# Interleaving the two layers of the expert stage, with the block loop written out for two blocks

## The chip, the cores and the metric

One core of one Trainium2 chip runs the whole program. The metric is the device time of one execution in microseconds (us). Engines: PE (TensorE matmuls; PEld its weight loads), DVE (VectorE), ACT (ScalarE), POOL (GpSimd), SP (SyncE). A name with q behind it (PEldq, DVEq, ACTq, POOLq) is the instruction sequencer of that engine, which does register work, branches and waits and hands the other instructions to the engine.

## The reference, cut to what matters

```
def _moe2_ref(x, modality_id, w_gate, modality_bias, w1, w2):
    logits = x @ w_gate + modality_bias[modality_id]
    e_idx = np.argmax(logits, axis=1)
    ...
    for e in range(E):                      # E = 8 experts, N = 3072 tokens, D = 512, F = 1024
        mask = e_idx == e
        h = np.maximum(x[mask] @ w1[e], 0.0)
        out[mask] = gate_w[mask, None] * (h @ w2[e])

def reference(...):
    attn_out = _attn_ref(q, k, v, n_sink, window)        # sink and window attention
    x = attn_out as (3072, 512)
    x = _moe_ref(x, w_in, w_out)                         # h = x @ w_in; (h - tanh(h)) @ w_out
    return _moe2_ref(x, ...)                             # the stage that is changed
```

## The kernel before

The program has two parts. The first, "front", does attention, the dense layer and the gate, writes the tokens to device memory (x2) and a table of slots per expert, and ends near 830 us. The second, "experts", is the one that is changed. It works on blocks of 128 tokens of one expert. A plan made on the chip gives the number of blocks (the data of this run make 25, numbered 0 to 24), the row of slots of each block, its turn (which expert of the order, row 1 of the table `meta`) and, in `meta_late`, at which block the weights of a next turn are looked over, scaled and split. Here only one such change of weights happens, in blocks 0 to 2.

Products are made in float16 with both factors split in a high and a low part, three products for each. A block j passes these steps; the line numbers are those of the profile.

- `load_slots`, `gather` (POOL, L1543, L1550): the slots of block j+2 and then its 128 rows of x, in one buffer `xg`, free again when block j+1 is transposed. A one-element addition on POOL (L97) carries their waits.
- `scale_x` (DVE L1562 to L1566, ACT L1569): a power-of-two scale for each token.
- `transpose_x` (PE L1577 into `xt_ps`, ACT L1582 to `xg_hi`, DVE L1585 to `xg_lo`).
- `hidden` (PE L1602): 8 f x 3 products x 4 k = 96 products of 128 columns into two banks `hid_ps`; the weights of the turn's parity are addressed through registers, computed line by line. Then ACT (L1611) `hid_hi`, DVE (L1614) `hid_lo`, for each half.
- `output` (PE L1646): 8 f x 3 = 24 products of 512 columns into `y_ps`; ACT (L1652) scales by `y_scale` (DVE L1629, L1632, after ACT's load of the slots, L1622); POOL (L1657) scatters `y` to the output.
- `look_ahead`, `scale_ahead`, `split_ahead`: the weights of the next turn. Each asks `meta_late` by a read into a register (`read`, L1499) and an If, on PE once for a block, on DVE four times, on ACT three times, also where there is nothing to do.

The order on each engine is the order of the calls in `iteration`. PE does hidden(j), the question of `scale_ahead`, the transposes of j+1, output(j). Blocks 0 and 1 are written out, and then one loop runs j from 2 to NB-1 = 37 and skips by an If what lies behind the last block.

Of the kernel before, what the change touches and what calls it, by code (L numbers as in the profile page):

```python
# [16 lines left out]
F32 = mybir.dt.float32  # L17
# [33 lines left out]
MB = NB + 2  # L51
# [1413 lines left out]
def experts(nc, dram, shared):  # L1465
# [5 lines left out]
    with ExitStack() as ctx:  # L1471
# [9 lines left out]
        xg_hi, xg_lo = (sb(n, [P, DM], F16) for n in ("xg_hi", "xg_lo"))  # L1481
        hid_hi, hid_lo = (sb(n, [P, FE], F16) for n in ("hid_hi", "hid_lo"))
        y_scale = sb("y_scale", [P, 1], F32)
# [4 lines left out]
        y_ps = ps("y_ps", [P, DM], F32)  # L1488
# [3 lines left out]
                 "hid_mm hid_hi hid_lo y_mm y_step y_set y_out scattered slot_y_in "  # L1492
# [33 lines left out]
        def split_ahead(E, eng, j, at, pieces):  # L1526
            if at is not None and E in ("act", "dve") and len(pieces):
                s = read(eng, 2, at, NE)
                with eng.If(s > 0):
                    eng.wait_ge(q["y_mm"], j)  # L1530
                    shared.split(E, eng, s, pieces)
# [21 lines left out]
        def scale_x(E, eng, j):  # L1553

            if E == "dve":
                step = chain(eng, q["x_step"], 4 * j)
                ts = eng.tensor_scalar
                eng.wait_ge(q["gathered"], 16 * (j + 1))
                need(eng, q["x_scaled"], j)
                if not (isinstance(j, int) and j < 2):  # L1560
                    eng.wait_ge(q["y_set"], j - 1)
# [4 lines left out]
                ts(column(x_undo, j % 2).bitcast(I32), x_exp[:], float(-EXP1), None, ALU.add).then_inc(q["x_set"], 1)  # L1566
# [4 lines left out]
        def transpose_x(E, eng, j):  # L1571

            if E == "pe":
                eng.wait_ge(q["x_scaled"], j + 1)
                need(eng, q["xt_lo"], j)
                for k in range(KD):
                    mm = eng.transpose(xt_ps[:, k * P:(k + 1) * P], xg[:, k * P:(k + 1) * P], ident[:])  # L1577
                mm.then_inc(q["xt_done"], 1)
            if E == "act":
                eng.wait_ge(q["xt_done"], j + 1)  # L1580
                need(eng, q["hid_mm"], 2 * j)
                eng.activation(xg_hi[:], xt_ps[:, :], ACT.Copy).then_inc(q["xt_hi"], 1)  # L1582
            if E == "dve":
                eng.wait_ge(q["xt_hi"], j + 1)
                eng.tensor_tensor(xg_lo[:], xt_ps[:, :], xg_hi[:], ALU.subtract).then_inc(q["xt_lo"], 1)  # L1585

        def hidden(E, eng, j, s):

            for c in range(2):
                if E == "pe":  # L1590
                    par = s % 2
                    if c == 0:
                        eng.wait_ge(q["xt_lo"], j + 1)
                    if not (isinstance(j, int) and j == 0):
                        eng.wait_ge(q["hid_lo"], 2 * j - 1 + c)
                    for f in range(4 * c, 4 * c + 4):
                        i = 0
                        for x, w in ((xg_lo, shared.hi), (xg_hi, shared.lo), (xg_hi, shared.hi)):
                            for k in range(KD):
                                if c == 0 and f == 0 and i < KD:  # L1600
                                    eng.wait_ge(shared.w_lo[k], s + 1)
                                mm = eng.matmul(hid_ps[c][:, (f - 4 * c) * P:(f - 4 * c + 1) * P],  # L1602
                                                shared.piece(w, k, par)[:, f * P:(f + 1) * P], x[:, k * P:(k + 1) * P],
                                                start=(i == 0), stop=(i == 3 * KD - 1))
                                i += 1
                    mm.then_inc(q["hid_mm"], 1)
                half = slice(c * 512, (c + 1) * 512)
                if E == "act":
                    eng.wait_ge(q["hid_mm"], 2 * j + c + 1)
                    need(eng, q["y_mm"], j)  # L1610
                    eng.activation(hid_hi[:, half], hid_ps[c][:, :], ACT.Relu).then_inc(q["hid_hi"], 1)  # L1611
                if E == "dve":
                    eng.wait_ge(q["hid_hi"], 2 * j + c + 1)
                    eng.scalar_tensor_tensor(hid_lo[:, half], hid_ps[c][:, :], 0.0, hid_hi[:, half], ALU.max, ALU.subtract)\  # L1614
                       .then_inc(q["hid_lo"], 1)
# [8 lines left out]
        def output_scale(E, eng, j, s):  # L1624

            if E == "dve":
                eng.wait_ge(q["slot_y_in"], 16 * (j + 1))
                need(eng, q["y_out"], j)
                eng.tensor_tensor(y_scale[:], slot_y[:, 1:2].bitcast(F32), column(x_undo, j % 2), ALU.mult)\  # L1629
                   .then_inc(q["y_step"], 1)  # L1630
                eng.wait_ge(q["y_step"], j + 1)
                eng.tensor_tensor(y_scale[:], y_scale[:], column(shared.undo, s), ALU.mult).then_inc(q["y_set"], 1)  # L1632

        def output(E, eng, j, s):

            if E == "pe":
                par = s % 2
                need(eng, q["y_out"], j)
                for f in range(KF):
                    if f % 4 == 0:  # L1640
                        eng.wait_ge(q["hid_lo"], 2 * j + f // 4 + 1)
                    if f % 2 == 0:
                        eng.wait_ge(shared.w_lo[KD + f // 2], s + 1)
                    for i, (l, w) in enumerate(((hid_lo, shared.hi), (hid_hi, shared.lo), (hid_hi, shared.hi))):
                        rhs = shared.piece(w, KD + f // 2, par)[:, (f % 2) * DM:(f % 2 + 1) * DM]
                        mm = eng.matmul(y_ps[:, :], l[:, f * P:(f + 1) * P], rhs, start=(f == 0 and i == 0),  # L1646
                                        stop=(f == KF - 1 and i == 2))
                mm.then_inc(q["y_mm"], 1)
            if E == "act":
                eng.wait_ge(q["y_mm"], j + 1)  # L1650
                eng.wait_ge(q["y_set"], j + 1)
                eng.activation(y[:], y_ps[:, :], ACT.Copy, scale=y_scale[:]).then_inc(q["y_out"], 1)  # L1652
            if E == "pool":
                eng.wait_ge(q["y_out"], j + 1)
# [6 lines left out]
        def iteration(E, eng, j, ago_1, ago_2):  # L1661

            turn = 0 if isinstance(j, int) and j == 0 else read(eng, 1, j, NE) if E in ("pe", "dve") else None
# [24 lines left out]
            if E == "pool":  # L1688
                load_slots(E, eng, j + 2)
                gather(E, eng, j + 2)  # L1690
                output(E, eng, j, turn)

        def program(E, eng):
# [13 lines left out]
            scale_x(E, eng, 0)  # L1707
            transpose_x(E, eng, 0)
# [4 lines left out]
            scale_x(E, eng, 1)  # L1713
# [6 lines left out]
            if E == "pool":  # L1720
                eng.wait_ge(q["gathered"], 16 * (last + 3))
                eng.wait_ge(q["scattered"], 16 * (last + 1))
# [76 lines left out]
```

## Time and profile before

| what | value |
|---|---|
| median of 3 runs | 1199.46 us (1196.58 to 1199.63) |
| the profiled execution | 1196.78 us, its span 1195.0 us |
| busy in the span | PE 1048.7, DVE 731.0, ACT 620.8, POOL 401.1 us |
| granted TensorE clock, mean over the span | 0.964 |

The span goes from the first to the last instruction of the profiled execution. PE is busy for 88% of it; ends of matmuls are modelled, so that the starts of neighbouring matmuls say more about their rate than the busy time does.

### The profile page before, as it was taken

What the parts mean: (1) busy time and instruction counts of PE and PEld (TensorE: products, weight loads), DVE (VectorE), ACT (ScalarE), POOL (GpSimd) and SP (SyncE); (2) the same over time, 40 slices, a digit from 0 to 9 for tenths busy, and PEclk for the clock granted to TensorE, in tenths of its full rate; (3) what the DMA queues carried; (4) which work ended last, traced back from release to release, by engine and by line L of the source; (5) the groups of instructions that cost most, each with busy time, mean ns of one, the idle gap of its engine ahead of it and who ended that gap; (6) DMA issues with size and microseconds to landing.
All of it is one profiled execution on the core that took longest, in us unless ns stands there. A gap on an engine that the chain in (4) does not pass through costs nothing. (4 is left out here: it accounts for less than half of the span.)

```text
span 1195.0 us, 27235 instructions
## 1 busy us (share of the span) xinstructions
PE 1048.7 (88%) x7844; PEld 684.4 (57%) x7845; DVE 731.0 (61%) x2392; ACT 620.8 (52%) x1422; POOL 401.1 (34%) x463
## 2 busy tenths in 40 slices
PE   1767898999999999999999999982699999999995
PEld 0534455665665665665665665541466667666763
DVE  6787977678878678878678655565462222222221
ACT  2776766666677666676666664451342222222221
POOL 4786774223254124254124211002232222222221
PEclk9968999999999999999999999996799999999998
DMA  9821112313212412212312100400411111011111
GB/s 295 262 66 32 33 45 68 95 32 65 57 32 39 137 32 50 73 32 36 87 32 37 54 2 10 159 1 27 168 44 37 43 36 44 27 44 35 44 35 34
DMA packets 24248, 74.18 MB, mean 62 GB/s; under 512 B 10016, under 2 KB 10016, under 8 KB 22624
## 3 DMA queue, kind: packets, MB, share of 16 engines
q1 hardware_dynamic: 14768, 59.66, 18.4%
q0 software_dynamic: 5792, 13.43, 3.5%
q8 instruction: 42, 0.69, 0.3%
q10 hardware_dynamic: 3600, 0.03, 0.2%
q14 instruction: 46, 0.38, 0.1%
HBM read 60.04 MB, written 13.33 MB: 61 GB/s over the span
## 5 line engine op out<-in xcount | busy, mean ns | idle before, releaser
L758 PE MATMUL acc<-w_out_all,g_hi 128*128 128x512 f16 x768 | 228.3, 379 | 0.0
L702 PE MATMUL h_ps<-xt_hi,w_in_all 128*128 128x384 f16 x1024 | 210.4, 328 | 16.3 <-DVE g_raw L723 16.3
L758 PE MATMUL acc<-w_out_all,g_lo 128*128 128x512 f16 x384 | 145.4, 379 | 3.2 <-DVE g_lo L743 1.7
L702 PEld LDWEIGHTS h_ps<-xt_hi,w_in_all 128*128 128x128 f16 x1024 | 97.6, 98 | 76.7 <-DVE g_raw L723 14.7
L590 ACT ACTIVATE pt_hi<-pt_ps 128x256 f16<-128x256 f32 (+2 forms) x224 | 83.4, 379 | 109.5 <-PE pt_ps L607 105.0
L97 POOL TENSOR_TENSOR tick<-tick 1x1 f32<-1x1 f32 x87 | 17.2, 198 | 349.9 <-DVE payload L878 113.5
L743 DVE SCALAR_TENSOR_TENSOR g_lo<-g_raw,batch_scale,g_hi 128x384 f16<-128x384 f32 x128 | 95.1, 743 | 33.1 <-ACT g_hi L733 30.7
L758 PEld LDWEIGHTS acc<-w_out_all,g_hi 128*128 128x128 f16 x768 | 74.9, 98 | 69.2
L714 ACT ACTIVATE g_raw<-h_ps,batch_scale 128x384 f32<-128x384 f32 x128 | 74.2, 579 | 75.0 <-PE h_ps L702 73.8
L594 DVE TENSOR_TENSOR pt_lo<-pt_ps,pt_hi 128x256 f16<-128x256 f32 (+2 forms) x224 | 94.3, 423 | 28.9 <-ACT pt_hi L590 27.5
L428 POOL TENSOR_TENSOR q_stack<-qk_raw,q_stack 64x768 f16<-64x768 f32 x31 | 50.8, 1638 | 165.6 <-ACT q_stack L424 165.6
L702 PE MATMUL h_ps<-xt_lo,w_in_all 128*128 128x384 f16 x512 | 105.5, 329 | 0.0
L571 ACT ACTIVATE normed<-probs,row_sum 128x260 f32<-128x260 f32 (+1 forms) x192 | 92.9, 484 | 19.7 <-DVE row_sum L566 19.6
L723 DVE SCALAR_TENSOR_TENSOR g_raw<-h_ps,batch_scale,g_raw 128x384 f32<-128x384 f32 x128 | 78.4, 612 | 39.8 <-ACT g_raw L714 38.7
L733 ACT ACTIVATE g_hi<-g_raw,batch_scale 128x384 f16<-128x384 f32 x128 | 78.0, 610 | 43.6 <-DVE g_raw L723 43.1
L1602 PE MATMUL hid_ps<-xg_hi,ew_lo 128*128 128x128 f16 x800 | 95.8, 219 | 0.0
L553 ACT ACTIVATE probs<-probs,neg_max 128x260 f32<-128x260 f32 (+1 forms) x192 | 92.7, 483 | 5.8 <-DVE neg_max L548 5.7
L428 POOL TENSOR_TENSOR kl_stack<-qk_raw,kh_stack 128x1048 f16<-128x1048 f32 (+1 forms) x31 | 60.1, 1939 | 99.1 <-ACT kh_stack L424 97.9
L607 PE MATMUL pt_ps<-ident,normed 128*128 128x128 f32 x352 | 74.1, 286 | 20.4 <-ACT normed L571 20.4
L1614 DVE SCALAR_TENSOR_TENSOR hid_lo<-hid_ps,hid_hi 128x512 f16<-128x512 f32 x50 | 34.3, 691 | 91.8 <-ACT hid_hi L1611 91.8
L548 DVE CUSTOM_DVE_ANT_0 probs<-s_ps,mask 128x260 f32<-128x260 f32 (+1 forms) x180 | 73.1, 406 | 23.7 <-issue 22.4
L1602 PE MATMUL hid_ps<-xg_lo,ew_hi 128*128 128x128 f16 x800 | 85.1, 222 | 1.5 <-DVE xg_lo L1585 1.5
(263 smaller groups left out, 2222.0 us busy)
## 6 DMA issues: line engine op xcount, KB each, us to landing
qk_raw<-in_qk SPq DMA_DIRECT2D x64, 454.0 KB, 6.1
raw<-in_w SPq DMA_DIRECT2D x16, 512.0 KB, 8.5
v_raw<-in_v SPq DMA_DIRECT2D x4, 1536.0 KB, 9.8
x_tokens<-x SPq DMA_DIRECT2D x24, 256.0 KB, 4.8
w_in_all<-in_w_in SPq DMA_DIRECT2D x4, 1024.0 KB, 13.0
w_out_all<-in_w_out SPq DMA_DIRECT2D x4, 1024.0 KB, 12.2
slot_g<-slots POOLq DMA_DIRECT2D x27, 1.0 KB, 2.0
xg<-x_tokens,slot_g POOLq DMA_INDIRECT x27, 3.4
```

The lines of the kernel that those rows point to most:

```text
L428: eng.tensor_tensor(lo, raw[half], hi[half], ALU.subtract).then_inc(q["conv_lo"], 1)
L553: eng.activation(probs[:, r, cols], probs[:, r, cols], ACT.Exp, bias=neg_max[:, r:r + 1], scale=-1.0, accum_out=row_sum[:, r:r + 1]).then_ ...
L571: eng.activation(normed[:, u % 6, cols], probs[:, r, cols], ACT.Copy, scale=row_sum[:, r:r + 1])\
L590: eng.activation(pt_hi[:, at, :], out, ACT.Copy).then_inc(q["pt_hi_done"], 1)
L594: eng.tensor_tensor(pt_lo[:, at, :], out, pt_hi[:, at, :], ALU.subtract).then_inc(q["pt_lo_done"], 1)
L702: mm = eng.matmul(h_ps, w16[0][:, f, x * DM + k * P:x * DM + (k + 1) * P], r[:, par, k, :], start=(i == 0), stop=(i == 3 * KD - 1))
L714: eng.activation(g_raw[:, f % 2, :], h_ps, ACT.Tanh, scale=batch_scale[:, b, 0:1]).then_inc(q["tanh_done"], 1)
L723: eng.scalar_tensor_tensor(g, h_ps, batch_scale[:, b, 0:1], g, ALU.mult, ALU.subtract).then_inc(q["g_done"], 1)
L733: eng.activation(g_hi[f % 2][:], g, ACT.Copy, scale=batch_scale[:, b, 1:2]).then_inc(q["g_hi_done"], 1)
L743: eng.scalar_tensor_tensor(g_lo[f % 2][:], g, batch_scale[:, b, 1:2], g_hi[f % 2][:], ALU.mult, ALU.subtract)\
L758: mm = eng.matmul(acc[t][:, :], l[f % 2][:, t * P:(t + 1) * P], w16[1][:, f, x * DM:(x + 1) * DM], start=(f == 0 and i == 0), stop=(f == N ...
L1602: mm = eng.matmul(hid_ps[c][:, (f - 4 * c) * P:(f - 4 * c + 1) * P], shared.piece(w, k, par)[:, f * P:(f + 1) * P], x[:, k * P:(k + 1) * P ...
```

## The change

Iteration j now makes hidden(j) and output(j-1) together: after each of the 24 products of 512 columns come 4 of the 96 small ones. The question of `scale_ahead` and the transposes of block j+1 come after the 14th of the 24. `y_ps`, `xg_hi` and `xg_lo` get a second buffer, `relu` of the second half of block j moves into iteration j+1, the scale of the output is made in two steps (`output_part`, and `output_scale` at the end of DVE's iteration), and `scale_x` of block j+1 comes at the start of iteration j instead of that of j+2 near its end. PE reads two turns for a block, that of j and that of j-1. The loop is written out for two blocks in an inner loop of four trips, inside an outer loop of five; a whole trip of the outer loop is skipped behind the last block. Block 0's first layer and the last block's second layer stand alone (`first_iteration`, `last_output`).

```
-MB = NB + 2
+MB = NB + 6
...
-        xg_hi, xg_lo = (sb(n, [P, DM], F16) for n in ("xg_hi", "xg_lo"))
+        xg_hi, xg_lo = ([sb(f"xg_{n}{i}", [P, DM], F16) for i in range(2)] for n in ("hi", "lo"))
...
-        y_ps = ps("y_ps", [P, DM], F32)
+        y_ps = [ps(f"y_ps{i}", [P, DM], F32) for i in range(2)]
...
+        def turn_of(eng, j):
+            return 0 if isinstance(j, int) and j == 0 else read(eng, 1, j, NE)
+
+        def products(eng, j, p, free, ago_1):
+
+            turn = turn_of(eng, j)
+            before = turn_of(eng, j - 1)
+            small = hidden_products(eng, j, p, turn)
+            for i, _ in enumerate(output_products(eng, j - 1, 1 - p, free, before)):
+                if i == 14:
+                    scale_ahead("pe", eng, ago_1)
+                    transpose_x("pe", eng, j + 1, 1 - p)
+                for _ in range(4):
+                    next(small)
+
+        def iteration(E, eng, j, p, ago_1, ago_2):
+
             if E == "pe":
-                hidden(E, eng, j, turn)
-                scale_ahead(E, eng, ago_1)
-                transpose_x(E, eng, j + 1)
-                output(E, eng, j, turn)
-            if E == "act":
-                hidden(E, eng, j, turn)
-                transpose_x(E, eng, j + 1)
-                load_slots_again(E, eng, j)
+                products(eng, j, p, 0 if ago_2 is None else j - 2, ago_1)
+            if E == "act":
+                relu(E, eng, j - 1, 1)
+                scale_x(E, eng, j + 1, 1 - p)
+                relu(E, eng, j, 0)
+                transpose_x(E, eng, j + 1, 1 - p)
+                load_slots_again(E, eng, j - 1)
                 split_ahead(E, eng, j, ago_2, range(KD, PIECES))
                 look_ahead(E, eng, j)
-                split_ahead(E, eng, j, ago_1, range(2))
-                output(E, eng, j, turn)
-                scale_x(E, eng, j + 2)
-                split_ahead(E, eng, j, ago_1, range(2, KD))
-            if E == "dve":
-                hidden(E, eng, j, turn)
-                transpose_x(E, eng, j + 1)
-                output_scale(E, eng, j, turn)
+                split_ahead(E, eng, j, ago_1, range(KD))
+                output(E, eng, j - 1, 1 - p)
+            if E == "dve":
+                relu(E, eng, j - 1, 1)
+                output_part(E, eng, j - 1, 1 - p, turn_of(eng, j - 1))
+                scale_x(E, eng, j + 1, 1 - p)
+                scale_ahead(E, eng, ago_1)
+                relu(E, eng, j, 0)
+                transpose_x(E, eng, j + 1, 1 - p)
                 split_ahead(E, eng, j, ago_2, range(KD, PIECES))
                 look_ahead(E, eng, j)
-                scale_ahead(E, eng, ago_1)
-                scale_x(E, eng, j + 2)
                 split_ahead(E, eng, j, ago_1, range(KD))
+                output_scale(E, eng, j - 1)
...
-            iteration(E, eng, 0, None, None)
-            iteration(E, eng, 1, 0, None)
-            with eng.Fori(2, NB) as j:
-                with eng.If(j <= last):
-                    iteration(E, eng, j, j - 1, j - 2)
...
+            first_iteration(E, eng)
+            iteration(E, eng, 1, 1, 0, None)
+            with eng.Fori(0, (NB + 5) // 8) as g:
+                with eng.If(8 * g + 2 <= last):
+                    with eng.Fori(4 * g + 1, 4 * g + 5) as i:
+                        j = 2 * i
+                        with eng.If(j <= last):
+                            iteration(E, eng, j, 0, j - 1, j - 2)
+                            with eng.If(j + 1 <= last):
+                                iteration(E, eng, j + 1, 1, j, j - 1)
+            last_output(E, eng, last)
```

## Rows read from the trace of the kernel before

**Rows 1.** The page: busy time of each engine; one instruction queue (packets, MB).

```profile
PE 1048.7 (88%) x7844; PEld 684.4 (57%) x7845; DVE 731.0 (61%) x2392; ACT 620.8 (52%) x1422; POOL 401.1 (34%) x463
...
q8 instruction: 42, 0.69, 0.3%
```

**Rows 2.** The chain that ended last, expert stage: start us, us, what.

```profile
856.23 7.04 PE y_ps L1646 x24
...
891.49 6.77 PE hid_ps L1602 x96
...
1037.08 6.50 PE hid_ps L1602 x96
1043.58 0.84 issue
1044.42 0.63 PE xt_ps L1577 x4
1045.05 5.18 PE y_ps L1646 x24
...
1169.13 6.59 PE hid_ps L1602 x96
```

**Rows 3.** Windows, PE alone, of one block's small products: stretch, length, busy (count), clock.

```profile
1050.05:1052.72 2.67, 2.67 (x49) 1.00 0.00 0
1052.98:1056.90 3.92, 3.82 (x47) 1.00 0.18 67
```

**Rows 4.** PE's sequencer by line, 1044.5 to 1057.7: count, ns min/median/max, first and last start.

```profile
L1646 PEldq FUSED_REGOPS  x8: 46/46/46, 1044.6 to 1046.6; - x8
L1717 PEldq COMPARE_BRANCH  x1: 208/208/208, 1046.9 to 1046.9; - x1
L1718 PEldq COMPARE_BRANCH  x1: 82/82/82, 1047.3 to 1047.3; - x1
L1499 PEldq TENSOR_LOAD <-meta x1: 297/297/297, 1047.6 to 1047.6; - x1
L1595 PEldq FUSED_REGOPS  x1: 42/42/42, 1048.3 to 1048.3; - x1
L1602 PEldq FUSED_REGOPS  x32: 46/46/94, 1048.5 to 1055.8; - x32
L1602 PEldq ALU_OP  x32: 32/32/32, 1049.0 to 1056.3; - x32
L1522 PEldq COMPARE_BRANCH  x1: 215/215/215, 1057.1 to 1057.1; - x1
```

**Rows 5.** Timeline of the block of rows 4 on ACT and DVE: start us, us, what [idle before].

```profile
1045.81 0.69 DVE L1585 TENSOR_TENSOR xg_lo<-xt_ps,xg_hi 128x512 f16<-128x512 f32 x1 [0.87 <-ACT xg_hi L1582]
...
1051.18 0.69 DVE L1562 TENSOR_REDUCE x_top<-xg 128x1 f32<-128x512 f32 x1 [2.85 <-issue]
...
1052.82 0.72 ACT L1569 ACTIVATE xg<-xg,x_scale 128x512 f32<-128x512 f32 x1 [1.87 <-DVE x_undo L1566]
```

**Rows 6.** The DMA answer of the whole span, issues: count, KB each, us to landing.

```profile
slot_g<-slots POOLq DMA_DIRECT2D x27, 1.0 KB, 2.0
xg<-x_tokens,slot_g POOLq DMA_INDIRECT x27, 3.4
...
out<-y,slot_y POOLq DMA_INDIRECT x25, 2.8
```

**Rows 7.** Timeline of the first blocks on DVE.

```profile
852.70 0.69 DVE L1562 TENSOR_REDUCE x_top<-xg 128x1 f32<-128x512 f32 x1 [8.15 <-DMA xg<-x_tokens,slot_g]
...
859.36 4.60 DVE L1319 TENSOR_REDUCE tops<-raw 128x1 f32<-128x1024 f32 x4 [0.68 <-issue]
...
880.41 4.94 DVE L1373 SCALAR_TENSOR_TENSOR ew_lo<-raw,ew_scale,ew_hi 128x1024 f32 x4 [0.95 <-issue]
```

**Rows 8.** The end: the last output and scatter.

```profile
1182.40 0.69 ACT L1652 ACTIVATE y<-y_ps,y_scale 128x512 f32<-128x512 f32 x1 [4.49 <-PE y_ps L1646]
...
1183.95 1.02 POOL L1657 DMA_INDIRECT out<-y,slot_y  x1 [0.60 <-issue]
```

**Rows 9.** DVE's sequencer at the loop's branch, 1176 to 1196.

```profile
L1717 DVEq COMPARE_BRANCH  x14: 50/56/56, 1185.7 to 1194.6; - x14
```

**Rows 10.** Windows, PE alone, around the first gap of the stage, with the granted clock.

```profile
852.40:854.90 2.50, 0.24 (x5) 1.00 0.36 138
854.90:856.20 1.30, 0.66 (x4) 1.00 0.01 0
856.20:857.50 1.30, 1.27 (x5) 0.69 0.01 0
857.50:858.50 1.00, 1.00 (x4) 0.50 0.39 58
```

**Rows 11.** The DMA answer from 1090 to 1120 us: all queues that moved anything.

```profile
q0 software_dynamic: 432, 1.25, 12.9%
q10 hardware_dynamic: 288, 0.00, 0.5%
```

More of the change, by code:

```diff
@@ L1580, in transpose_x @@
                 eng.wait_ge(q["xt_done"], j + 1)
-                need(eng, q["hid_mm"], 2 * j)
-                eng.activation(xg_hi[:], xt_ps[:, :], ACT.Copy).then_inc(q["xt_hi"], 1)
+                if not (isinstance(j, int) and j < 2):
+                    eng.wait_ge(q["hid_mm"], 2 * j - 2)
+                eng.activation(xg_hi[p][:], xt_ps[:, :], ACT.Copy).then_inc(q["xt_hi"], 1)
             if E == "dve":
                 eng.wait_ge(q["xt_hi"], j + 1)
-                eng.tensor_tensor(xg_lo[:], xt_ps[:, :], xg_hi[:], ALU.subtract).then_inc(q["xt_lo"], 1)
@@ L1587, in hidden, with hidden_products @@
-        def hidden(E, eng, j, s):
+                eng.tensor_tensor(xg_lo[p][:], xt_ps[:, :], xg_hi[p][:], ALU.subtract).then_inc(q["xt_lo"], 1)
+        def hidden_products(eng, j, p, s):
+            par = s % 2
+            eng.wait_ge(q["xt_lo"], j + 1)
             for c in range(2):
[L1590 to L1607, printed above, removed]
-                if E == "act":
-                    eng.wait_ge(q["hid_mm"], 2 * j + c + 1)
-                    need(eng, q["y_mm"], j)
-                    eng.activation(hid_hi[:, half], hid_ps[c][:, :], ACT.Relu).then_inc(q["hid_hi"], 1)
-                if E == "dve":
-                    eng.wait_ge(q["hid_hi"], 2 * j + c + 1)
-                    eng.scalar_tensor_tensor(hid_lo[:, half], hid_ps[c][:, :], 0.0, hid_hi[:, half], ALU.max, ALU.subtract)\
-                       .then_inc(q["hid_lo"], 1)
@@ new lines, in hidden_products @@
+                if not (isinstance(j, int) and j == 0):
+                    eng.wait_ge(q["hid_lo"], 2 * j - 1 + c)
+                for f in range(4 * c, 4 * c + 4):
+                    i = 0
+                    for x, w in ((xg_lo, shared.hi), (xg_hi, shared.lo), (xg_hi, shared.hi)):
+                        for k in range(KD):
+                            if f == 0 and i < KD:
+                                eng.wait_ge(shared.w_lo[k], s + 1)
+                            mm = eng.matmul(hid_ps[c][:, (f - 4 * c) * P:(f - 4 * c + 1) * P],
+                                            shared.piece(w, k, par)[:, f * P:(f + 1) * P], x[p][:, k * P:(k + 1) * P],
+                                            start=(i == 0), stop=(i == 3 * KD - 1))
+                            i += 1
+                            if f == 4 * c + 3 and i == 3 * KD:
+                                mm.then_inc(q["hid_mm"], 1)
+                            yield
@@ new lines, in relu @@
+        def relu(E, eng, j, c):
+            half = slice(c * 512, (c + 1) * 512)
+            if E == "act":
+                eng.wait_ge(q["hid_mm"], 2 * j + c + 1)
+                need(eng, q["y_mm" if c else "y_half"], j)
+                eng.activation(hid_hi[:, half], hid_ps[c][:, :], ACT.Relu).then_inc(q["hid_hi"], 1)
+            if E == "dve":
+                eng.wait_ge(q["hid_hi"], 2 * j + c + 1)
+                eng.scalar_tensor_tensor(hid_lo[:, half], hid_ps[c][:, :], 0.0, hid_hi[:, half], ALU.max, ALU.subtract)\
+                   .then_inc(q["hid_lo"], 1)
@@ L1622, in load_slots_again, with output_part, output_scale @@
                 eng.dma_start(slot_y[:], dram["slots"][bass.ds(row, P), :]).then_inc(q["slot_y_in"], 16)
-        def output_scale(E, eng, j, s):
+        def output_part(E, eng, j, p, s):
+            if E == "dve":
+                need(eng, q["y_set"], j)
+                eng.tensor_tensor(y_part[:], column(x_undo, p), column(shared.undo, s), ALU.mult).then_inc(q["y_part_set"], 1)
+        def output_scale(E, eng, j):
             if E == "dve":
                 eng.wait_ge(q["slot_y_in"], 16 * (j + 1))
[L1628 to L1648, printed above, removed]
+                eng.wait_ge(q["y_out"], j + 1)
@@ new lines, in output_scale, with output_products @@
+                eng.wait_ge(q["y_part_set"], j + 1)
+                eng.tensor_tensor(y_scale[:], slot_y[:, 1:2].bitcast(F32), y_part[:], ALU.mult).then_inc(q["y_set"], 1)
+        def output_products(eng, j, bank, free, s):
+            par = s % 2
+            eng.wait_ge(q["y_out"], free + 1)
+            for f in range(KF):
+                if f % 4 == 0:
+                    eng.wait_ge(q["hid_lo"], 2 * j + f // 4 + 1)
+                if f % 2 == 0:
+                    eng.wait_ge(shared.w_lo[KD + f // 2], s + 1)
+                for i, (l, w) in enumerate(((hid_lo, shared.hi), (hid_hi, shared.lo), (hid_hi, shared.hi))):
+                    rhs = shared.piece(w, KD + f // 2, par)[:, (f % 2) * DM:(f % 2 + 1) * DM]
+                    mm = eng.matmul(y_ps[bank][:, :], l[:, f * P:(f + 1) * P], rhs, start=(f == 0 and i == 0),
+                                    stop=(f == KF - 1 and i == 2))
+                    if i == 2 and f in (3, KF - 1):
+                        mm.then_inc(q["y_half" if f == 3 else "y_mm"], 1)
+                    yield
@@ L1649, in output @@
+        def output(E, eng, j, bank):
             if E == "act":
@@ L1651, in output @@
                 eng.wait_ge(q["y_set"], j + 1)
-                eng.activation(y[:], y_ps[:, :], ACT.Copy, scale=y_scale[:]).then_inc(q["y_out"], 1)
+                eng.activation(y[:], y_ps[bank][:, :], ACT.Copy, scale=y_scale[:]).then_inc(q["y_out"], 1)
             if E == "pool":
-                eng.wait_ge(q["y_out"], j + 1)
+                eng.wait_ge(q["y_out"], j + 2)
                 carry_waits(eng, tick, 3, q["carried_3"], j)
@@ L1690, in iteration, with first_iteration, last_output @@
                 gather(E, eng, j + 2)
-                output(E, eng, j, turn)
+                output(E, eng, j - 1, 1 - p)
+        def first_iteration(E, eng):
+            if E == "pe":
+                for _ in hidden_products(eng, 0, 0, 0):
+                    pass
+                transpose_x(E, eng, 1, 1)
+            if E in ("act", "dve"):
+                scale_x(E, eng, 1, 1)
+                relu(E, eng, 0, 0)
+                transpose_x(E, eng, 1, 1)
+                look_ahead(E, eng, 0)
+            if E == "pool":
+                load_slots(E, eng, 2)
+                gather(E, eng, 2)
+        def last_output(E, eng, last):
+            if E == "pe":
+                for _ in output_products(eng, last, 0, last, turn_of(eng, last)):
+                    pass
+            if E == "act":
+                relu(E, eng, last, 1)
+                load_slots_again(E, eng, last)
+                output(E, eng, last, 0)
+            if E == "dve":
+                relu(E, eng, last, 1)
+                output_part(E, eng, last, last % 2, turn_of(eng, last))
+                output_scale(E, eng, last)
+            if E == "pool":
+                output(E, eng, last, 0)
+                eng.wait_ge(q["gathered"], 16 * (last + 3))
+                eng.wait_ge(q["scattered"], 16 * (last + 1))
         def program(E, eng):
```

25 lines of the change are left out of this document (11 added, 14 removed).

## Prediction

> **What bounds the kernel now.** I read the page first: PE is the busiest engine with 1048.7 of 1195.0 us, 7844 matmuls [rows 1]. That does not say that the array is the limit, so I went on to the chain that ended last, restricted to the stage that is changed. From hidden(3) at 891.49 to hidden(24) at 1169.13 it repeats one pattern: 6.5 to 6.6 us small products, 0.84 "issue", 0.63 transposes, 5.18 large products [rows 2]. From 891.49 to 1169.13 are 21 blocks, so 13.22 us a block. No wait for DVE, ACT or a DMA sets a step of it. Whoever reads only this sees a PE with one hole of 0.84 us.
>
> The second reading is the rate inside the 6.6 us. The first 48 small products of a block start 2.67 us apart, 56 ns each; the other 47 to 48 take 3.92 us, 83 ns each, at the same granted clock of 1.00 [rows 3]. The same instruction at the same clock in two rates: the second rate is not the array's. So what feeds the array? The third view is PE's sequencer by line over one period [rows 4]. Its register work for the large products runs from 1044.6 to 1046.6, for the small ones from 1048.5 to 1056.3: 8 f in 7.9 us, 0.99 us for 12 products, 83 ns each, also from 1048.5 to 1050.05, when the array is still behind with the large ones. Each f carries 4 FUSED_REGOPS of 46 and 4 ALU_OP of 32 ns, 0.31 of the 0.99 us. Put end to end over a period:
>
> - issue of 24 large products, 1044.6 to 1046.8: 2.2
> - the loop's branch and If, to the read: 0.6 (208 and 82 ns with what lies between)
> - the read of the turn, to 1048.3 (load of 297 ns, address and bounds work): 0.9, and 0.2 to the first small product
> - issue of 96 small products, to 1056.4: 7.9
> - the question of `scale_ahead` (branch of 215 ns at 1057.1), to 1057.5: 1.1
> - transposes, to 1057.8: 0.3
>
> The sum is 13.2, the whole period. PE's sequencer has no free time in a block. It runs 3.3 us ahead of the array in the large products (which start 216 ns apart but are issued in 90), spends 1.7 of that in the loop head, and the rest carries the first 48 small ones. The array's own need is 96 x 56 ns + 5.18 + 0.63 = 11.2 us; the other 2.0 us are the sequencer's.
>
> **The change part by part.** *Interleaving.* It moves 120 products and their 80 register operations; it removes none. Four small and one large product are issued in 5 x 83 = 0.42 us and take 4 x 56 + 216 = 0.44 us on the array: well balanced, and worth 13.2 - 11.2 = 2.0 us a block if the sequencer had the time. It has not: saved array time turns into a longer empty stretch where the sequencer is in the loop head. I cost the interleaving at 0. Bounds: -2.0 if I misread who sets the pace, 0 otherwise.
>
> *A second turn on PE* (`before`): 0.9 us as today's read [rows 4], and 0.1 for its parity and wait count. Nothing hides it, since all on that sequencer is in series. Bounds: 0.65 (the read in `scale_ahead`, 1056.4 to 1057.1, without branch) and 1.1.
>
> *Loop for two blocks.* The head of 0.6 is paid once for two blocks, and a second If (82 ns, some 0.15 with its sum) comes to it: -0.2 a block. The outer loop costs about a head more in 8 blocks, +0.1. Expressions of 2i in waits: 0 to 0.1.
>
> So +0.9 us a block (0.5 to 1.2): 14.1 instead of 13.2. For 21 blocks, 4 to 24: +19 (10 to 25).
>
> *Do the other engines keep up?* The new ring goes: transposes, `xg_hi`, `xg_lo` (ends 1.45 us after the transposes, 1046.50 against 1045.05), three reads on DVE (2.85 by the idle time before L1562), `output_scale` 0.2, ACT's output 0.7, ACT's loop head and relu 1.1, `hid_lo` 0.7, DVE's turn and `output_part` 1.1, `scale_x` from 1051.18 to ACT's end at 1053.54, 2.4, transposes 0.8 [rows 5]. Sum 11.3 us, under 14.1, so it costs nothing; it would become the bound if PE came under 11.3. The gather of 3.4 and slots of 2.0 us [rows 6] have their iteration as before. The scatter (2.8) must land before the slots are loaded again; both lie in the first 10 us of the iteration. The larger MB lengthens some ten plan operations by 36 elements, 0.3 us in all.
>
> *Start, blocks 0 to 3.* Today relu(0) waits for `scale_x(1)`, whose rows land at 852.70; the splits end at 885.4 [rows 7]. In the new order `look_ahead(0)` (4.6 us) stands before relu of block 0's second half, so `hid_lo` comes at 863.4 and `scale_x(2)` ends at 867 with the transposes behind it (some 2 us stall); the scales of the weights come after them, the four splits of 1.28 us end at about 878, hidden(2) waits for them (3 us), and `output_scale` behind the second four splits makes block 3 late by 1.6. Before, nearly all of this lay under PE's own work. I take +7; bounds 0 (all covered) and +10.
>
> *End.* The last output ends at 1183.1, the scatter is issued at 1183.95 and lands 2.8 later [rows 6, 8]: about 1187. But the span ends at 1195.0, since DVE still goes through 13 skipped blocks, 1185.7 to 1194.6, 0.69 us each [rows 9]. The change leaves two skipped outer trips (1.4 us) and they lie beside PE's last large products. From the end of hidden(24): exits and the last turn 2.5, 24 large products 5.2, output 0.9, issue 0.9, landing 2.8, 0.2: 12.5 instead of 1195.0 - 1175.7 = 19.3: -7 (-8 to -5).
>
> Sum: +19 +7 -7 = +19 us on the profiled execution of 1196.8, so 1216; the median of the runs stands 2.7 above that execution, and so I say 1218 for the median. What measurement can tell is about 0.3%, 3.6 us.
>
> **The rivals.** *Array-bound (0.15, faster).* If the slow 83 ns were weight loads that only a wide product can hide, interleaving would hide them and PE would need 11.2; then DVE's ring of 11.3 binds: 21 x -1.9 = -40, with start and end 1159 to 1162. For it: 98-ns loads, and PE busy 88%. Against it: 48 products in a row at 56 ns without any wide product between [rows 3], and register work that paces evenly in both halves [rows 4]. It decides if the sequencer can issue a block in under 13 us. The Trainium skill, "TensorE: Matmul & The Clock Gate", section "Back-to-back issue gap", gives a stream of load and product pairs about 81 ns at 128 and 131 ns at 512 columns, set by both together. By that rule a block would need 96 x 81 + 24 x 131 ns, 10.9 us and transposes, an estimate of 11.5 us in any order; the trace disagrees with it in both numbers (56, and 216 at 512), and agrees only where the sequencer has register work.
>
> *No difference (0.10).* The read costs 0.65, expressions nothing, loop savings more, and the start is covered: 21 x 0.4 - 7 = about +1, 1197 to 1203.
>
> *The clock (0.08, slower).* The empty stretch on the array grows from 0.84 to some 2.3 us a block. Once a gap like it stood before 854.94, and the clock fell to 0.50 after it [rows 10]; the large products took 7.04 for 5.18, 1.9 us lost [rows 2]. At every block: 23 x 1.9 = 43 more, 1261. Against it: the array has 2.9 us a block to spare, so a fall must cost more than that before it reaches the sequencer; and that gap had a second one of 0.63 behind it.
>
> *Fetching the loop's code (0.07, slower).* The loop on PE goes from some 350 to some 730 instructions. Today no instruction queue moves anything in the loop [rows 11]; all 42 packets make 0.69 MB [rows 1], 16 KB each. If the longer loop did not stay, each of 12 trips would wait for one fetch of at least 2.0 us, the shortest landing [rows 6]: +24, 1242; with three packets +72. The Trainium skill, "Runtime: NRT & Kernel Launch", section "Instruction fetch mechanics", says that a branch to a page outside the window waits for a fetch, and gives PE room for 2048 instructions; no run here shows either.
>
> **How the numbers follow.** Forecast 0.60: slower, 1206 to 1228 (the bounds +10 to +25, 0 to +10, -8 to -5, not all at once). The rest as above. Range 1196 to 1242: it leaves out most of the faster case and the far ends of the two slow ones, 0.2 together. Slower by over 0.3%: 0.60 + 0.08 + 0.07 = 0.75; within: 0.10; faster: 0.15.
>
> **What the new profile would show.** PE's sequencer: two TENSOR_LOADs of `meta` a block and no free time in a period of about 14.1; small products in groups of four between wide ones, a hole of 2 us at the head of each block and a smaller one at the transposes; ACT, DVE and POOL waiting for PE. Output L1652 waits for `y_ps` or for `y_scale` by under 1 us. At the end one or two skipped trips, 12 to 13 us from the last small product to the end. No packets of q8 in the loop. I am wrong if the period is under 13.2, above all if the sequencer's register work is then spaced closer than 0.99 us for an f, or if PE's transposes wait for `xg` in every block (the ring is longer than I think).

## The result and the profile after

The changed kernel takes 1210.39 us (median of 4 runs, 1207.58 to 1214.46) against 1198.42 us of the kernel before on the same chip (4 runs, 1196.58 to 1199.63). The ratio is 1.0104, with a 95% interval of 1.0068 to 1.014: slower by 1%, small but clear of the spread between executions. The profiled execution took 1212.05 us with a span of 1210.5, against 1196.78 and 1195.0 before. It lies 1.7 above its median and the one of before 1.6 below its own, so the two spans differ by 15.5 us and the medians by 12.0. What follows divides the 15.5.

The page: busy time of each engine, share and instructions; the group of the large products, with the idle time before it.

```profile
PE 1043.0 (86%) x7844; PEld 675.2 (56%) x7845; DVE 729.6 (60%) x2387; ACT 618.8 (51%) x1421; POOL 398.0 (33%) x463
...
L1654 PE MATMUL y_ps<-ew_hi,hid_lo 128*128 (+1 forms) x200 | 77.8, 389 | 32.2 <-ACT y L1665 16.2
```

PE makes the same 7844 products and is busy for 5.7 us less than in [rows 1], in a span that is 15.5 us longer: the new time is time in which the array has nothing to do. The page puts 16.2 us of it down to ACT's `y`. The chain takes that up and shows the period (start us, us, what):

```profile
901.33 0.69 ACT y L1665
...
1036.95 0.63 PE xt_ps L1578 x4
...
1041.57 0.69 ACT y L1665
1042.27 0.97 issue
...
1051.05 0.63 PE xt_ps L1578 x4
...
1064.44 0.63 PE xt_ps L1578 x4
...
1193.84 0.69 ACT y L1665
```

From `y` at 901.33 to `y` at 1193.84 are 21 blocks: 292.5 us, 13.93 each, where [rows 2] give 13.22. The transposes stand 14.10 us apart over the head of the inner loop (1036.95 to 1051.05) and 13.39 where only the inner If lies between (to 1064.44). The 0.69 of `y` and the 0.97 behind it span the array's hole at the start of a block. In the timeline of PE (start, us, what, [idle before]):

```profile
1041.16 0.38 PE L1654 MATMUL y_ps<-ew_hi,hid_hi 128*128 x1
1041.37 0.39 PE L1602 MATMUL hid_ps<-xg_hi,ew_hi 128*128 128x128 f16 x4
1043.24 0.39 PE L1654 MATMUL y_ps<-ew_hi,hid_lo 128*128 x1 [1.48 <-ACT y L1665]
```

Small and large products alternate, as they should. The first one of the new block stands behind 1.48 us of nothing. Its buffer is two blocks old, so it need not wait for the `y` that happens to end there; what its sequencer does in that time is the next view. PE's sequencer by line over two blocks, 27.5 us (count: ns min/median/max, first and last start):

```profile
L1500 PEldq TENSOR_LOAD <-meta x5: 300/304/309, 1027.5 to 1055.0; - x5
L1602 PEldq FUSED_REGOPS  x64: 46/46/96, 1029.4 to 1054.1; - x64
L1654 PEldq FUSED_REGOPS  x16: 46/46/108, 1029.0 to 1053.6; - x16
L1779 PEldq COMPARE_BRANCH  x1: 207/207/207, 1040.7 to 1040.7; - x1
```

The register work is that of [rows 4]: 64 FUSED_REGOPS for two blocks of L1602, 32 each, and 8 each for the large products. The loop branch (0.21) comes once for two blocks. A turn is loaded four times for two blocks where it was loaded twice; the fifth record, at 1055.0, belongs to the next pair. The register work of a block ends at 1040.7 with the loop branch, and the array runs dry 1.0 us later.

### The profile page after: what moved, and what is told of

Its sections match the earlier page's. It is cut to its first block and busy times, and to the rows that moved or that the text cites. A ratio compares the mean times of both kernels' runs of the same rounds, so it can differ in the third digit from the quotient of the medians.

```text
span 1210.5 us, 26838 instructions
## 1 busy us (share of the span) xinstructions
PE 1043.0 (86%) x7844; PEld 675.2 (56%) x7845; DVE 729.6 (60%) x2387; ACT 618.8 (51%) x1421; POOL 398.0 (33%) x463
## 5 line engine op out<-in xcount | busy, mean ns | idle before, releaser
L1654 PE MATMUL y_ps<-ew_hi,hid_lo 128*128 (+1 forms) x200 | 77.8, 389 | 32.2 <-ACT y L1665 16.2
L1602 PE MATMUL hid_ps<-xg_lo,ew_hi 128*128 128x128 f16 x800 | 85.2, 224 | 3.3 <-DVE xg_lo L1587 2.2
```

What stands on the lines that cost most here:

```text
L1654: mm = eng.matmul(y_ps[bank][:, :], l[:, f * P:(f + 1) * P], rhs, start=(f == 0 and i == 0), stop=(f == KF - 1 and i == 2))
```

## The experiments

Medians in us; each ratio is to the kernel before on the same chip: 1198.42 us for the changed kernel, 1197.65 for e1 to e4, 1197.73 for e5 to e8. Where kernels of different groups are compared below, these 0.8 us are part of the difference. "Period" is the mean over the 21 blocks of the loop, or the usual length of the two kinds of block.

| kernel | median | ratio, 95% interval | period of a block |
|---|---|---|---|
| before | 1198.42 | 1 | 13.22 |
| after | 1210.39 | 1.0104 (1.0068 to 1.014) | 13.93 |
| e1: after, fixed weight buffer | 1164.6 | 0.9735 (0.9716 to 0.9754) | 12.1 and 11.26 |
| e2: after, not interleaved | 1228.69 | 1.0263 (1.0246 to 1.028) | 14.11 |
| e3: after, second read taken out of every other block | 1203.57 | 1.0064 (1.0041 to 1.0087) | 14.1 and 12.62 |
| e4: before, with a second read | 1214.99 | 1.0141 (1.012 to 1.0161) | 13.97 |
| e5: before, fixed weight buffer | 1154.04 | 0.9627 (0.9593 to 0.9662) | 11.32 |
| e6: before, complete, If on the turn's parity | 1157.67 | 0.9653 (0.9617 to 0.9689) | 11.51 |
| e7: before, with the two-level loop alone | 1193.35 | 0.9956 (0.9939 to 0.9974) | 13.27 |
| e8: e6 and e7 together | 1154.55 | 0.9629 (0.9594 to 0.9664) | 11.51 |

Theory 1 is that of the prediction: PE's sequencer works through a block in series, and the array follows it. The rival is that the array, or the way products and weight loads follow each other on it, sets the rate.

**e1 and e5: take the register work away.** The weights lie in two buffers by the parity of the turn, which is in a register. With a constant for the parity the 80 register operations a block are gone, and every product and load remains. These two kernels use the weights of buffer 0 for all blocks, so they leave the choice of the right expert out.

```
-            par = s % 2
+            par = 0
```

> The changed kernel, but PE takes the expert weights of both layers always from the first of the two buffers, so their addresses are constants and the 80 register operations of a block that compute them are gone; the blocks of the second expert are multiplied with the first expert's weights (the output is not the reference's). Theory 1 (PE's sequencer sets the block: 13.9 us of register work, reads and branches in series): the sequencer loses some 8 us a block, the array (11.2 us) or the ring over ACT and DVE (11.3 us) becomes the bound, period 11.2 to 12, 1210 - 21 x 2.0 to 2.7 = 1153 to 1168 us. Theory 2 (the array is slowed by weight loads or by the mix of widths, not by register work): nothing in a load or product is changed, so 1206 to 1214 us. Theory 3 (the new waits between ACT, DVE and PE hold PE): also unchanged, 1206 to 1214 us.

> The kernel before with the weights of both layers always from the first of the two buffers on PE (constant addresses, no register operation for them; the second expert's blocks are multiplied with the first expert's weights). Theory 1 (sequencer): with its 8 us a block of register work gone the order of before, too, is bound by the array's 11.2 us or by DVE's row of waits, 11.2 to 12.0 us a block: 1198 - 23 x 1.2 to 2.0 = 1152 to 1170 us, no later than the same edit on the changed kernel (1164.6). If interleaving were what the array needs to run at full rate, this would stay above 1180 us.

e1 took 1164.6 and e5 1154.04 us. Timeline of PE in e1, two neighbouring transposes:

```profile
1047.21 0.60 PE L1578 MATMUL xt_ps<-ident,xg 128*128 128x128 f32 x4
...
1058.47 0.60 PE L1578 MATMUL xt_ps<-ident,xg 128*128 128x128 f32 x4
```

They stand 11.26 us apart. The chain of e5:

```profile
1044.08 0.63 PE xt_ps L1577 x4
1044.70 5.18 PE y_ps L1646 x24
1049.88 5.36 PE hid_ps L1602 x96
1055.24 0.11 issue
1055.35 0.63 PE xt_ps L1577 x4
```

The 96 small products that took 6.50 to 6.77 us in [rows 2] take 5.36, 56 ns each for all 96, and the hole of 0.84 is 0.11. This is the array's own 11.2 us, in the old order. The rival falls: nothing of the order of products, of loads or of shapes was changed in e5, only register work. Nothing is left there for an interleaving to win. e1 stands 10.6 us above e5; it differs from it in the order, the second read, the loop and the work of the other engines together, so that the 10.6 are not the price of the order alone. Part of them is a hole of 0.83 us that the array still has at each loop head in e1, where a block takes 12.1. PE's sequencer takes the loop branch at 1038.4 and the array has work until 1039.9; in e5 the branch is at 1046.0 and the large products last until 1049.9. In both some 17 or 18 products are then still to be worked off, by a count of the products in the timeline; where they are large ones they cover 3.9 us of the loop head, where small and large alternate 1.5. What limits the lead to that number is not shown.

The timeline of PE in the kernel before has one more sign of the cause, inside the slow half of its small products:

```profile
1054.01 0.58 PE L1602 MATMUL hid_ps<-xg_hi,ew_lo 128*128 128x128 f16 x4
1054.43 0.39 PE L1602 MATMUL hid_ps<-xg_hi,ew_hi 128*128 128x128 f16 x4
1054.66 0.45 PE L1602 MATMUL hid_ps<-xg_lo,ew_hi 128*128 128x128 f16 x4
1054.99 0.60 PE L1602 MATMUL hid_ps<-xg_hi,ew_lo 128*128 128x128 f16 x4
```

The last four products of an f (`xg_hi`, `ew_hi`) use the four addresses that its first four (`xg_lo`, `ew_hi`) used, so by the code they need no new address. They take 0.23 us, near the 56 ns a product of the fast half; the four before them take 0.42 and the first four of the next f 0.33. The 83 ns of [rows 3] are a mean of these.

**e4 and e3: the second read alone.** e4 puts an unused read into the old kernel, e3 takes it out of the second block of each pair of the new one, where the turn of the block before is still in a register.

```
             if E == "pe":
+                if not isinstance(j, int):
+                    read(eng, 1, j - 1, NE)
                 hidden(E, eng, j, turn)
```

```
-            before = turn_of(eng, j - 1)
+            before = carried["turn"] if p and not isinstance(j, int) else turn_of(eng, j - 1)
+            carried["turn"] = turn
```

> The kernel before with one more read of a turn on PE in each block of the loop (its value is not used), nothing else. Theory 1: 23 blocks x 0.75 us = +17 us, 1214 to 1218 us, the period 13.2 becomes 13.95. Theory 2 (the read is hidden behind the array's backlog of large products): 0 to +3 us, 1198 to 1202 us.

> The changed kernel, but in the second half of the two-block loop PE takes the turn of block j-1 from the register that the first half read, instead of reading it again. Theory 1: one read of 0.75 us (by the sequencer's records of the changed kernel) less in every second block, 11 or 12 times in all: 8 to 9 us faster than the changed kernel, 1201 to 1203 us. If the reads lie beside the array's work (theory 2), no change: 1208 to 1212 us.

PE's sequencer in e4, reads of `meta` in one block:

```profile
L1499 PEldq TENSOR_LOAD <-meta x2: 304/309/314, 1047.1 to 1047.9; - x2
```

The two loads start 0.8 us apart; the period is 13.97, 0.76 above the 13.21 of before by the same count, and 23 x 0.76 = 17.5 is the 17.3 that the medians differ by. In e3 the second blocks went from 13.4 to 12.62 us, 0.78 for a read again. Its median lies 6.8 us under that of the changed kernel (6.1 when each is taken against its own kernel before), where 8 to 9 was expected. In its profile the clock fell five times in the 21 blocks, near 893, 982, 1036, 1091 and 1145, at 0.5 to 1.0 us each, against two falls in the profile of the changed kernel. That can account for the rest; a run with the clock held would be needed to show it.

**e7: the two-level loop alone.** The old kernel, its loop written as in the change.

```
-MB = NB + 2
+MB = NB + 6
...
-            with eng.Fori(2, NB) as j:
-                with eng.If(j <= last):
-                    iteration(E, eng, j, j - 1, j - 2)
+            with eng.Fori(0, (NB + 5) // 8) as g:
+                with eng.If(8 * g + 2 <= last):
+                    with eng.Fori(4 * g + 1, 4 * g + 5) as i:
+                        j = 2 * i
+                        with eng.If(j <= last):
+                            iteration(E, eng, j, j - 1, j - 2)
+                            with eng.If(j + 1 <= last):
+                                iteration(E, eng, j + 1, j, j - 1)
```

> The kernel before with only the loop of the change: written out for two blocks, inner loop of four trips in an outer loop that skips whole trips; order, buffers and the one read of a turn as before. Theory 1: a quarter of a microsecond a block less in the head, some 0.7 us more for each of 3 outer trips, so 23 x -0.2 + 2 = -3; at the end 13 skipped blocks of 0.69 us on DVE become two skipped trips, and the last scatter's landing and POOL's drain of 2.3 us set the end instead: -4 to -5. Together 1188 to 1193 us. If the longer loop has to be fetched again at each trip: above 1200 us.

1193.35 us, 4.4 under before, just above the 1188 to 1193 that was expected. The chain shows why:

```profile
1042.84 0.63 PE xt_ps L1577 x4
...
1056.05 0.63 PE xt_ps L1577 x4
...
1069.17 0.63 PE xt_ps L1577 x4
```

13.21 and 13.12 us; over the whole loop such neighbours add up to 26.4, twice the old 13.21, and a trip of the outer loop costs 0.7 more. Writing the loop out saves nothing in the loop. What it gives is the end: from the last transposes to the end of the span are 12.8 us (1188.70 to 1201.5), 18.4 before (1176.56 to 1195.0). -5.6 there, 21 x 0.06 = +1.2 in the loop and +0.2 in blocks 0 to 3 are -4.2 of the 4.4. This profile is of an execution of 1203.13 us, 9.8 above the median of its kernel; its stage starts 10.7 us later than in the profile of before (first transposes at 852.78 and 842.07), ahead of all that was changed, and the stretches above are counted from there on.

**e2: the interleaving alone undone.** The new kernel, its small products all before the large ones.

```
-            small = hidden_products(eng, j, p, turn)
+            for _ in hidden_products(eng, j, p, turn):
+                pass
...
-                for _ in range(4):
-                    next(small)
```

> The changed kernel with its two-block loop, two turn reads, second buffers and orders on the other engines, but PE makes the 96 small products of block j first and then the 24 large ones of block j-1: the interleaving alone is undone. Theory 1 (sequencer in series): the same instructions, so the same 13.9 us a block, 1207 to 1214 us. Theory 2 (interleaving is worth something on the array, the 2.0 us between 13.2 and 11.2, and something else ate it): 21 to 23 x up to 2.0 us longer, 1215 to 1250 us. Theory 3 (interleaving itself hurts, by breaking the order of loads): faster, towards 1198 us.

This missed: 1228.69 us, where theory 1 allowed no more than 1214; the time lies in the range of the rival, 1215 to 1250, which would have it from blocks that are up to 2.0 us longer. They are not: the steady part has 14.11 a block, 0.18 above the interleaved kernel and 3.8 in 21 blocks (0.28 where the two falls of the clock in the changed kernel are left out). Why a sequencer in series gains even that by the order is not shown. Most of the rest is in blocks 1 and 2, where the transposes stand 19.93 and 20.22 us apart instead of 14.60 and 14.74. The chain of e2 there:

```profile
876.02 1.16 ACT ew_hi L1369
877.49 0.77 DVE ew_lo L1373
...
882.28 0.16 DVE y_scale L1641
...
883.18 0.60 ACT hid_hi L1616
883.81 0.70 DVE hid_lo L1619
884.65 4.93 PE hid_ps L1602 x48
```

Before PE's first small products of the block, at 884.65, stand ACT's and DVE's splits of the next expert's weights, then `y_scale` behind them on DVE, and only then `hid_hi` and `hid_lo`. So interleaving has a worth of its own: with the weights' splits on ACT and DVE it saves some 11 us in these two blocks. Not all of that is hidden waiting: behind each of the two empty stretches the granted clock was down (windows of PE: a mean of 0.61 from 885 to 890, 0.50 from 903 to 908), and the 48 small products took 4.93 and 5.14 us where 47 take 3.92 at 1.00 [rows 3], so some 1 us a block is the clock's. But the splits stand in ACT's and DVE's new order, which the interleaving asked for; in the order of before they were largely covered without it (13.29 and 14.79 us between the transposes around blocks 2 and 3).

**e6 and e8: the register work out, the kernel whole.** The cause points to a repair: ask the parity once by an If, and write the products out with constant buffers behind it. e6 does this in the kernel before, e8 with the loop of e7 as well.

```
...
+                odd = turn % 2
+                with eng.If(odd > 0):
+                    hidden(E, eng, j, turn, 1)
+                with eng.If(odd < 1):
+                    hidden(E, eng, j, turn, 0)
                 scale_ahead(E, eng, ago_1)
                 transpose_x(E, eng, j + 1)
+                with eng.If(odd > 0):
+                    output(E, eng, j, turn, 1)
+                with eng.If(odd < 1):
+                    output(E, eng, j, turn, 0)
```

> The kernel before, complete and correct, with each layer on PE written twice, once for each weight buffer with constant addresses, and an If on the turn's parity in front of each. Theory 1: the 80 register operations of a block go, four Ifs (two taken through, two skipped, 0.08 and 0.21 us each) come, together some 0.6 to 1.0 us of a sequencer that now has over 5 us free: 11.2 to 12.3 us a block, 1152 to 1177 us. Theory 2 (register work is not the bound): 1198 to 1220 us.

> The kernel before, complete and correct, with both: the two layers written twice behind Ifs on the parity, and the two-level loop for two blocks. Theory 1: the head saving no longer counts where the array is the bound, the tail saving of 4 to 5 us does: 2 to 8 us under the kernel with the Ifs alone, 1146 to 1172 us. The loop on PE now has some 1100 instructions: if its length matters, it is slower than the kernel with the Ifs alone.

1157.67 and 1154.55 us: 3.5% and 3.7% under before. The two lie 0.3% apart, about what can be told here, and as expected. The chain of e8:

```profile
1048.55 0.36 issue
1048.91 0.65 PE xt_ps L1577 x4
1049.56 5.18 PE y_ps L1646 x24
1054.74 5.36 PE hid_ps L1602 x96
```

It is the chain of e5 with 0.36 "issue" for 0.11 in this block. No order of products was touched, and it is 4.6% under the change (1154.55 to 1210.39).

## Why the prediction came out, step by step

The direction and the mechanism were right, and the total came near; that it did is in part luck. Of the three terms, +19, +7 and -7, the first was somewhat too large and the other two were both wrong, by 6.1 us too much and 4.4 us too little, so that they nearly cancel. Another 2.2 us of the measured 15.5 are not the change's.

| stretch | predicted | measured, span |
|---|---|---|
| up to the first transposes of the stage | 0 | +2.18 |
| from there to the end of the small products of block 3 | +7 | +0.89 |
| 21 blocks of the loop | +19 | +15.05 |
| from the end of the small products of block 24 | -7 | -2.62 |
| sum | +19 | +15.50 |

The marks are, before, the ends of the small products of blocks 3 and 24, 898.26 and 1175.72, and after, the starts of `y` at 901.33 and 1193.84.

**The start of the stage** is not the change's. The first transposes are at 842.07 before and at 844.25 after. In other profiles, with the same work ahead of it, it stood at 840.9 (e1), 841.2 (e3), 844.5 (e2), 846.7 (e4) and 852.8 (e7). It belongs to the spread between executions, and goes some way to explain why the spans differ by more than the medians.

**The loop's term, +19: right in kind, mis-sized.** It was put at +0.9 a block, made of "a second turn on PE" 1.0, "loop for two blocks" -0.2 and +0.1, and "interleaving" 0. The period grew by 0.72, from 13.21 to 13.93. The read measured 0.76 (e4) and 0.78 (e3); 0.9 had been taken, with 0.65 as the lower bound. The loop for two blocks gave nothing: 13.27 against 13.21 in e7, and 14.11 in e2 against 13.97 in e4, both with two reads and no interleaving, is +0.14, half of it two outer trips of 0.7; e2 also has the new buffers and the new order on ACT and DVE, so the rest may be theirs. The interleaving was costed at 0 and gave -0.18 (e2 to after). The steps 0.76 + 0.14 - 0.18 make 0.72 because they lead from before over e4 and e2 to after; they are no check of each other. That the read costs its whole length is the statement "PE's sequencer has no free time in a block", and e4 shows it by itself.

**"The array's own need is 11.2 us; the other 2.0 are the sequencer's"**: shown by e5, 11.32, and by the shorter blocks of e1, 11.26. The first evidence for it, 56 and 83 ns of the same product [rows 3], held: without register work all 96 take 5.36 us.

**The start, +7: the step that failed** is "hidden(2) waits for them", the splits. It took for granted that block 2 already uses the next expert's weights. The data give their tokens to two experts only, 1550 and 1522 of them, 13 and 12 blocks; so what is split in blocks 1 and 2 is used first at the 14th. I had the sizes of the splits from the profile [rows 7] and not the table of the turns. What they do cost is a shorter chain, seen in the changed kernel too:

```profile
870.68 1.16 ACT ew_hi L1369
872.15 0.77 DVE ew_lo L1373
...
877.84 0.60 ACT hid_hi L1616
...
881.11 0.73 ACT xg L1570
881.97 0.64 PE xt_ps L1578 x4
...
896.71 0.63 PE xt_ps L1578 x4
```

The splits hold up the relu (`hid_hi`) and, behind it, the scaling of `xg` and the transposes. From 881.97 to 896.71 are 14.74 us where a block without the loop head takes 13.4, so 1.3 more; from 867.37 to 881.97, over the entry of the loop, are 14.60, where a block with an outer trip takes 14.8, so nothing. That is little; PE has products of both blocks to issue meanwhile, and e2 shows what it is when it has not. The stall of 2 us at the transposes of block 2 did not come either: PE is busy without a gap from 860 to 872.

**The end, -7: two things missed.** Timeline of PE, ACT and POOL at the end of the changed kernel, and POOL's sequencer after it:

```profile
1196.46 0.39 PE L1654 MATMUL y_ps<-ew_hi,hid_lo 128*128 x1 [2.44 <-issue]
...
1203.54 0.69 ACT L1665 ACTIVATE y<-y_ps,y_scale 128x512 f32<-128x512 f32 x1 [7.23 <-PE y_ps L1654]
...
1205.08 1.02 POOL L1670 DMA_INDIRECT out<-y,slot_y  x1 [0.58 <-issue]
```

```profile
L1787 POOLq DRAIN  x1: 2263/2263/2263, 1208.0 to 1208.0; - x1
```

Issue to landing is the forecast 2.8, to 1207.8; then POOL drains for 2.26 us more. Before, the same 2.26 us began at 1190.0 and lay beside DVE's skipped blocks [rows 9]. And the last large products do not take 5.2 us: from 1196.46 to `y` at 1203.54 are 7.1. Windows of PE (stretch, length, busy (count), clock):

```profile
1196.00:1198.00 2.00, 1.54 (x7) 0.90 0.36 135
1198.00:1200.00 2.00, 2.00 (x6) 0.50 0.07 9
```

After the 2.44 us gap of the last turn's read and the exits the granted clock goes to 0.50, the lower of its two levels (1.2 GHz), while the large products run: 1.9 us, the same loss as in [rows 2, 10]. 2.3 and 1.9 make 4.2: that is what lies between the forecast 12.5 and the 16.7 measured. That DVE's skipping shrinks was right: its sequencer passes the outer loop's branch three times, the last at 1195.4, in place of 14.

**The rivals.** *Array-bound* is refuted by e5 and e6, in which the array reaches 11.3 and 11.5 a block without interleaving. The Trainium skill, "TensorE: Matmul & The Clock Gate", section "Back-to-back issue gap", gives 81 ns at 128 and 131 ns at 512 columns for pairs of load and product. The trace disagrees with both: in e5, 5.36 us for 96 is 56 ns and 5.18 for 24 is 216. 83 ns, which looks like its figure, went away with the register work.

*The clock* was real and small. Windows of PE in the changed kernel's loop:

```profile
1010.00:1014.00 4.00, 3.26 (x39) 1.00 0.26 66
1014.00:1017.00 3.00, 2.12 (x16) 0.95 0.22 87
1017.00:1020.00 3.00, 3.00 (x19) 0.50 0.01 0
```

It fell to 0.50 behind 7 us in which the array stood idle for 0.74 and 0.88, and the block took 15.1 instead of 14.1 (from 1008.45 to 1023.54). This happened twice in 21 blocks (near 904 and 1017), not at all in those of before, and five times in e3. The gap of 1.5 us is in every other block; why it is followed by a fall in these and not in the others stays open. It is part of the 15.1: 2 x 1.0. The times of the changed kernel spread over 6.9 us, and its slower runs have the lower mean clock: 1207.58 and 1208.74 us at 0.967 and 0.968, 1212.05 and 1214.46 at 0.962 and 0.963. Falls in varying number would do that, but they need not lie in the loop: the 13 runs of before beside e5 to e8 spread over 9.5 us in the same way, from 1195.16 at 0.969 to 1204.69 at 0.962.

*Fetching the loop's code* did not come. DMA queues from 905 to 1180 in the changed kernel (packets, MB, share):

```profile
q0 software_dynamic: 3771, 10.03, 11.5%
q10 hardware_dynamic: 2880, 0.02, 0.5%
```

No instruction queue moves anything. e8, with PE's products written out four times in its loop, has one instruction packet between 905 and 1000 and none from 1000 to 1142. The Trainium skill, "Runtime: NRT & Kernel Launch", section "Instruction fetch mechanics", gives PE room for 2048 instructions; the trace agrees as far as it goes.

*No difference* had two of its parts: the start was covered, and the read cost little more than 0.65. It would have needed the end's -7 as well.

*Do the other engines keep up?* They do, behind block 3. Waits in the changed kernel, 900 to 1190 (who waits, for whom: us, times, longest):

```profile
ACT y L1665 <- PE y_ps L1654: 68.6, 21, 3.3
...
PEld y_ps L1654 <- issue: 30.3, 21, 2.3
```

ACT waits up to 3.3 us for PE in each block; PE's own loads wait for "issue", 1.4 a block, and for no other engine. The ring of 11.3 us never showed: e1 came to 11.26 in its shorter blocks, about the same, and to 12.1 in the others, so nothing here tells whether the array or the ring bound it there.

## What to carry to other kernels

When one instruction has two rates at one clock, look at the engine's sequencer before reordering its work. Addresses from a register cost the sequencer for every change of address, and a value with few states is better asked once by a branch, with constant addresses behind it: 3.5% here, where reordering for the array's sake lost 1%. Before costing a wait, look up in the data when the awaited thing is first used; and when a tail is cut off one engine, look for what it covered on the others.

## What the runs showed of the hardware

Eight register operations and 12 products take PE's sequencer 0.99 us in the kernel before. If all of it is put down to the operations, that is 0.12 us each, some three times their records of 32 and 46 ns. That pairs of load and product cost it little beside them is read from one place: the last ALU_OP of one f starts at 1050.4 and the first FUSED_REGOPS of the next at 1050.5, and by the code four products with their loads lie between them. e5 gives only a bound, 56 ns a pair, at which the array is full. With the operations gone a block is 1.9 us shorter (13.21 to 11.32), which is what the array allows and not what the sequencer saved. A branch that jumps back took 0.21 us on PE, one that falls through 0.08 (76 ns on L1783, the inner If). POOL needed 2.26 us to drain after its last indirect DMA had landed, in the kernel before and in the changed one. PE's sequencer stood 17 to 18 products ahead of the array at the loop head of e1 and e5.
